# Gathering the sink columns on VectorE instead of ScalarE, in the attention stage of a fused kernel

## The chip, the core and the metric

The kernel runs on one NeuronCore of a Trainium2 chip. The metric is the device time of one execution in microseconds (us). The engines are TensorE (PE in the profile, its weight loads PEld), VectorE (DVE), ScalarE (ACT), GpSimd (POOL) and SyncE (SP), which issues the transfers. Each runs its own list of instructions in order, and they wait for each other by semaphores.

## What is computed

Three layers in a row, for 2 sequences of 768 positions. The change touches the first alone: attention of 16 heads (2 x 8) with a window of 128 positions and 4 "sink" positions that every query may see.

```python
scores = scale * np.matmul(q, k.transpose(0, 1, 3, 2))        # 2 x 8 heads, 768 x 768, D = 64
is_sink = pos[None, :] < int(n_sink)                            # 4
rel = pos[:, None] - pos[None, :]
in_window = (rel >= 0) & (rel < int(window))                    # 128
scores = np.where(is_sink | in_window, scores, -1000000000.0)
a = np.exp(scores - np.max(scores, axis=-1, keepdims=True))
a = a / (np.sum(a, axis=-1, keepdims=True) + 1e-09)
return np.matmul(a, v)
```

Behind it come a causal attention of four experts of which two count for each position, and a gated layer with a mix over the positions. They follow when all heads are done.

## The kernel before

A head's 768 queries are T = 6 tiles of 128. A query tile t sees the key tile before it, its own, and the 4 sinks, so its scores are one tile of WIN = 260 columns: 128, then 4 sinks, then 128 (for t = 0 only the last 132). The 16 heads use two sets of buffers in turn (s = 0 for even heads, 1 for odd). In one "step" of a head, `pe_step`, `act_step` and `dve_step` each do the later half of the work of that head and the first half of the next head's. The loops of the engines hold two steps, one for each s; heads 0 and 1 and the last two stand outside of them. I call the place between the two steps the middle of the body, and the place where the loop turns its edge.

First half, for head + 1 in the step of head: TensorE scores a tile (`score_tile`, two matmuls with kS as keys and qH, qL as queries); VectorE adds the mask, scales and takes the row minimum of the negated scores (`mask_tile`, SM and NM, one custom instruction and a short one that reads its accumulator); ScalarE takes the exponential and its row sum (`exp_tile`, Pa and RS). SM has a ring of three, so a mask waits for the exponential three tiles back.

Second half, for head: TensorE turns Pa in three groups (`turn_group`); ScalarE copies groups 0 and 2 out of PSUM and VectorE group 1 (`copy_group`, PTa); TensorE multiplies them by va (`weigh_group`). The sink columns go another way: `gather_sinks` copies the 4 sink columns of all six tiles, out of Pa, three times into one tile `sinks` of 128 x 96 (72 columns are written), TensorE turns that (`turn_sinks`), VectorE writes it to PS in a rounded and a rest part (`copy_sinks`), and TensorE multiplies PS by vs (`weigh_sinks`), which ends the head's sum. Then VectorE adds epsilon to the row sums and inverts them (`invert_sums`, a TENSOR_SCALAR and a RECIPROCAL on RI, 128 x 6), and in the next step multiplies the head's sum by them (`normalise`, X).

The gather before is ScalarE's, behind the last exponential of a head and ahead of the copy of group 0 in the next step. TensorE's order in a step is: score 0, turn group 0, score 1, turn group 1, turn the sinks, score 2, turn group 2, weigh group 0, scores 3 and 4, weigh group 1, score 5, weigh group 2, weigh the sinks.

GpSimd works beside them, once a pair of heads for each: it splits the queries of a later head (`split_queries`: qH, then qL, which waits for qH), lays out the sinks' values (`lay_out_sinks`: vs, which waits for `weigh_sinks` of an earlier head), and splits a strip of weights for the next layer (`split_strip`: wbH, then wbL). In the order of its loop: qH and qL of the even head, vs of the even head, qH and qL of the odd head, wbH and wbL, vs of the odd head. So the vs that follows an even step, in the middle of the body, has qH, qL, wbH and wbL behind it, and the vs that follows an odd step, at the edge, has qH and qL of the next turn. SyncE loads keys, queries and values a pair ahead.

Of the kernel before, what the change touches and what calls it, by code (L numbers as in the profile page):

```python
# [19 lines left out]
ACT = mybir.ActivationFunctionType  # L20
# [3 lines left out]
P = 128  # L24
B, H, S, D = 2, 8, 768, 64
T = S // P
SINK, WINDOW = 4, 128
# [12 lines left out]
BLK = P + SINK  # L40
# [58 lines left out]
def fused_attention_experts_gated(nc, qT, kT, v, vsink, vdiag, w_b, w_in, g_ln, w_sgT, b_sg, w_out, out):  # L99
    ctx = ExitStack()  # L100
    with ctx:
        def sb(name, shape, dt=F32, stack=ctx):
            return stack.enter_context(nc.sbuf_tensor(name, shape, dt))

        def sem(name):
            return ctx.enter_context(nc.semaphore(name))
# [26 lines left out]
        with ExitStack() as st:  # L133
# [5 lines left out]
            Pa = [sb(f"Pa{s}", [P, T, WIN], F32, st) for s in range(2)]  # L139
            SM = [sb(f"SM{s}", [P, WIN], F32, st) for s in range(RING)]  # L140
            PTa = [sb(f"PTa{s}", [P, BANK], F32, st) for s in range(2)]
            sinks = [sb(f"sinks{s}", [P, SROWS], F32, st) for s in range(2)]
# [24 lines left out]
        with ExitStack() as st:  # L167
# [14 lines left out]
        s_ = {n: sem(n) for n in (  # L182

            "consts", "pool_step",

            "q_split", "k_high", "k_split", "scored", "masked", "expd", "turned", "turned_in_act", "turned_in_dve",
            "sinks_gathered", "sinks_turned", "sinks_high", "sinks_in", "sv_in", "sv_high", "sv_low", "vs_ready",
            "weighed", "summed", "x_ready", "dve_step", "wb_split", "wo_split", "dve_chain",

            "dve_tick", "pool_tick",  # L190
# [194 lines left out]
        def _(act):  # L385
# [7 lines left out]
            def exp_tile(s, head, t, again):  # L393
                n = T * head + t
                act.wait_ge(s_["masked"], n + 1)
                if again and t == 0:
                    act.wait_ge(s_["turned"], GROUPS * (head - 1))
                    act.wait_ge(s_["sinks_gathered"], head - 1)
                    act.wait_ge(s_["dve_step"], 2 * head - 3)
                a = P if t == 0 else 0  # L400
                nc.scalar.activation(Pa[s][:, t, a:WIN], SM[t % RING][:, a:WIN], ACT.Exp, bias=NM[:, s, t:t + 1], scale=-1.0,  # L401
                                     accum_out=RS[:, s, t:t + 1]).then_inc(s_["expd"], 1)

            def gather_sinks(s, head, again):

                act.wait_ge(s_["expd"], T * (head + 1))
                if again:
                    act.wait_ge(s_["sinks_turned"], head - 1)
                nc.scalar.activation(sinks[s][:, :].rearrange("p (k n) -> p k n", k=3)[:, :, 0:T * SINK].rearrange("p k (t c) -> p k t c", t=T),
                                     Pa[s][:, :, P:BLK].unsqueeze(1).broadcast_to((P, 3, T, SINK)), ACT.Copy)\  # L410
                    .then_inc(s_["sinks_gathered"], 1)

            def copy_group(s, head, g, again):
                act.wait_ge(s_["turned"], GROUPS * head + g + 1)
                if again or g:
                    act.wait_ge(s_["weighed"], GROUPS * head + g - 1)
                m, a = (s + g) % 2, P if g == 0 else 0
                nc.scalar.activation(PTa[m][:, a:], banks[:, 4 + m, a:], ACT.Copy).then_inc(s_["turned_in_act"], 1)

            def x_high(b, t):  # L420

                act.wait_ge(s_["x_turned"], T * b + t + 1)
                nc.scalar.activation(xH[:, :, t * P:(t + 1) * P], banks[:, X_BANKS[t % RING], :].rearrange("p (k n) -> p k n", k=KT),
                                     ACT.Copy).then_inc(s_["x_high"], 1)

            def act_step(s, head, again, keys, nxt):

                copy_group(s, head, 0, again)
                for t in range(T):
                    if nxt:  # L430
                        exp_tile(1 - s, head + 1, t, again or s)
                    else:
                        x_high(0, t)
                    if t == 0 and keys is not None:
                        high_keys(s, head + 2, keys, True)
                    if t == 2:
                        copy_group(s, head, 2, again)
                if nxt:
                    gather_sinks(1 - s, head + 1, again or s)

            high_keys(0, 0, 0, False)
            high_keys(1, 1, 0, False)
            for t in range(T):
# [1 line left out]
                    act.wait_ge(s_["sv_in"], 32)  # L445
                    nc.scalar.activation(sv[:, :], sv_raw[:, :], ACT.Copy).then_inc(s_["sv_high"], 1)
                exp_tile(0, 0, t, False)
            gather_sinks(0, 0, False)
            act_step(0, 0, False, 1, True)
            act_step(1, 1, True, 1, True)  # L450
            with act.Fori(1, PAIRS - 1) as i:
# [28 lines left out]
            for b in range(B):  # L480
                for n, (kind, j, g) in enumerate(PROJ_ORDER):
                    wait("projected", PROJ * b + n + 1)
                    c = slice(g * G3 * P, (g + 1) * G3 * P)
# [37 lines left out]
            for b in range(B):  # L521
                for t in range(T):
                    n = T * b + t
# [11 lines left out]
                for t in range(T):  # L535
                    n = T * b + t
# [9 lines left out]
        def _(dve):  # L546
# [21 lines left out]
            def copy_group(s, head, again):  # L568
# [3 lines left out]
                m = (s + 1) % 2  # L572
                nc.vector.tensor_copy(PTa[m][:, :], banks[:, 4 + m, :]).then_inc(s_["turned_in_dve"], 1)  # L573

            def copy_sinks(head, again):
                dve.wait_ge(s_["sinks_turned"], head + 1)
                if again:
                    dve.wait_ge(s_["summed"], head)
                nc.vector.tensor_copy(PS[:, :], banks[0:SROWS, 2, 0:P]).then_inc(s_["sinks_high"], 1)
                dve.wait_ge(s_["sinks_high"], head + 1)  # L580
                low = slice(64, 64 + T * SINK)
                nc.vector.tensor_tensor(PS[low, :], banks[low, 2, 0:P], PS[low, :].bitcast(F32), ALU.subtract)\
                    .then_inc(s_["sinks_in"], 1)
# [9 lines left out]
            def normalise(s, head, turn):  # L593
                dve.wait_ge(s_["dve_step"], 2 * head + 2)
                dve.wait_ge(s_["summed"], head + 1)
                at = bass.ds(turn * T * P, T * P)
                nc.vector.tensor_tensor(X[:, at].rearrange("p (t n) -> p t n", t=T)[:, :, s * D:(s + 1) * D],
                                        banks[:, 6 + s, 0:T * D].rearrange("p (t d) -> p t d", t=T),
                                        RI[:, :].unsqueeze(2).broadcast_to((P, T, D)), ALU.mult).then_inc(s_["x_ready"], 1)
# [9 lines left out]
            def dve_step(s, head, before, again, keys, nxt):  # L609

                for t in range(T):
                    if nxt:
                        mask_tile(1 - s, head + 1, t, True)
                    if t == 0 and before is not None:
                        normalise(1 - s, head - 1, before)
                    if t == 2:
                        copy_group(s, head, again)
                    if t == 2 and keys:
                        low_keys(s, head + 2)
                    if t == 3:  # L620
                        copy_sinks(head, again)
                    if not nxt:
                        x_low(0, t)
                invert_sums(s, head, again)
# [101 lines left out]
            for b in range(B):  # L726
                for n, (kind, j, g) in enumerate(PROJ_ORDER):
                    if kind == "kq":
                        wait("proj_high", PROJ * b + n + 1)
                        c = slice(g * G3 * P, (g + 1) * G3 * P)  # L730
# [43 lines left out]
            for b in range(B):  # L774
# [4 lines left out]
                for t in range(T):  # L779
                    n = T * b + t  # L780
# [25 lines left out]
                for t in range(T):  # L806
                    n = T * b + t
# [362 lines left out]
```

## Time and profile before

| | us |
|---|---|
| median of 3 runs | 448.91 (448.79 to 448.92) |
| the profiled execution | 448.91, of which the span of the trace is 446.7 |
| busy in the span: PE, PEld | 418.4, 368.7 |
| busy: DVE, ACT, POOL | 269.4, 211.1, 130.2 |
| mean granted clock of TensorE | 0.992 of full speed |

The attention stage fills about the first 120 us of the span, the rest belongs to the other two layers. "Busy" is the time for which an instruction's record is open, so an instruction that stands and waits for something inside itself counts as busy. The records are given as start and length in us from the span's start; a line number such as L589 is that of the kernel printed above. "Idle before" and its releaser stand in brackets at the end of a row where an engine waited.

### The profile page before, as it was taken

To read this page: it belongs to the slowest core of one execution; us is meant where nothing else is said; L and a number is where in the kernel's file an instruction comes from. 1 tells how busy PE (TensorE), PEld (TensorE's weight loads), DVE (VectorE), ACT (ScalarE), POOL (GpSimd) and SP (SyncE) were. 2 spreads that over 40 slices of the span, in tenths; PEclk is the share of its full clock that TensorE was granted. 3 is DMA by queue.
4 is the path that set the end of the run, shared out by engine and by line. 5 is a ranking of instruction groups with operands and counts; after the bars stand their busy time and mean duration, and the time that the engine had idled before them with its cause. 6 is when DMAs were issued, how large, how long until landed. Compare 5 with 4: busy or idle time off the path is not lost.

```text
span 446.7 us, 8137 instructions
## 1 busy us (share of the span) xinstructions
PE 418.4 (94%) x2608; PEld 368.7 (83%) x2608; DVE 269.4 (60%) x687; ACT 211.1 (47%) x545; POOL 130.2 (29%) x144
## 2 busy tenths in 40 slices
PE   0899899989999999989998998999999999999997
PEld 0787788878999999869997997888888888888885
DVE  0899999999838775640879653277423335652322
ACT  2777777787646655444774653434210114331010
POOL 7877676685673000000037400232000000000000
PEclk9999999999999999989999998999999999999999
DMA  8876576571432000000003300100001010000011
GB/s 192 200 198 155 143 186 172 144 183 46 122 104 73 0 1 2 0 1 1 0 25 104 87 1 0 25 24 1 0 0 49 23 72 0 1 0 0 30 42 70
DMA packets 14156, 27.72 MB, mean 62 GB/s; under 512 B 2256, under 2 KB 5328, under 8 KB 14128
## 3 DMA queue, kind: packets, MB, share of 16 engines
q1 hardware_dynamic: 14128, 27.35, 23.1%
q8 instruction: 17, 0.28, 0.3%
q14 instruction: 11, 0.09, 0.1%
HBM read 24.20 MB, written 3.15 MB: 61 GB/s over the span
## 4 chain that ended last, share of the span: by engine, by line
PE 74%; DVE 10%; issue 7%; ACT 6%; DMA 1%; POOL 1%; DVEq 0%; SPq 0%; ACTq 0%; POOLq 0%
PE banks L826 13%; PE banks L828 13%; PE banks L827 13%; PE banks L1098 11%; PE banks L1000 7%; PE banks L978 4%; PE banks L989 4%; ACT Pa L401 3%; PE banks L877 3%; DVE kS L553 3%; DVE RI L589 2%; DVE SM L564 2%; PE banks L841 2%; PE banks L857 2%; PE banks L892 1%
## 5 line engine op out<-in xcount | busy, mean ns | idle before, releaser
L401 ACT ACTIVATE Pa<-SM,NM 128x260 f32<-128x260 f32 (+1 forms) x96 | 46.7, 487 | 22.8 <-DVE NM L564 22.4
L877 PE MATMUL banks<-va,PTa 128*128 128x64 f32 x352 | 46.0, 272 | 3.8 <-DVE PTa L573 3.3
L877 PEld LDWEIGHTS banks<-va,PTa 128*128 128x128 f32 x352 | 43.1, 191 | 6.5 <-DVE PTa L573 6.5
L841 PE MATMUL banks<-kS,qH 128*128 128x260 f32 x96 | 34.8, 367 | 13.2 <-POOL qL L321 10.8
L1000 PE MATMUL banks<-vg,PTb 128*128 128x64 f32 x336 | 44.6, 267 | 1.0 <-DVE Y L679 1.0
L1000 PEld LDWEIGHTS banks<-vg,PTb 128*128 128x128 f32 x336 | 42.2, 191 | 1.9 <-issue 1.4
L470 ACT ACTIVATE Pb<-Pb,NM 128x128 f32<-128x128 f32 (+5 forms) x48 | 31.9, 664 | 22.3 <-DVE NM L665 22.1
L564 DVE CUSTOM_DVE_ANT_0 SM<-banks,win 128x260 f32<-128x260 f32 (+1 forms) x96 | 36.4, 403 | 6.2 <-PE banks L841 3.4
L539 ACT ACTIVATE gH<-banks 128x512 fp32r<-128x512 f32 x12 | 7.2, 600 | 68.4 <-PE banks L1118 68.4
L826 PE MATMUL banks<-w_inH,x2H 128*128 128x512 f32 x96 | 38.1, 397 | 0.0
L828 PE MATMUL banks<-w_inH,x2L 128*128 128x512 f32 x96 | 37.5, 391 | 0.0
L827 PE MATMUL banks<-w_inL,x2H 128*128 128x512 f32 x96 | 37.4, 390 | 0.0
L374 POOL TENSOR_TENSOR rstd<-vare,minus_half 128x1 f32<-128x1 f32 x12 | 6.6, 553 | 98.7 <-DVE vare L787 98.7
L665 DVE CUSTOM_DVE_ANT_0 Pb<-banks,causal 128x128 f32<-128x128 f32 (+5 forms) x48 | 29.4, 620 | 7.6 <-PE banks L978 7.4
L841 PEld LDWEIGHTS banks<-kS,qH 128*128 128x128 f32 x96 | 19.1, 199 | 17.1 <-issue 10.5
L321 POOL TENSOR_TENSOR qL<-qd,qH 128x768 fp32r<-128x768 f32 x16 | 31.3, 1958 | 1.3
L796 DVE SCALAR_TENSOR_TENSOR Gd<-banks,b_all,U 128x512 f32<-128x512 f32 x12 | 9.0, 751 | 37.2 <-PE banks L1098 37.2
L360 POOL TENSOR_SCALAR w_sgH_first<-raw 128x512 fp32r<-128x512 f32 x6 | 3.7, 622 | 94.3 <-PE banks L828 92.0
L989 PE MATMUL banks<-ident,Pb 128*128 128x128 f32 x168 | 29.7, 278 | 0.9 <-ACT Pb L470 0.6
L1098 PE MATMUL banks<-vnH,w_sgL 128*128 128x512 f32 x72 | 28.3, 393 | 0.0
L857 PE MATMUL banks<-ident,Pa 128*128 128x128 f32 x176 | 27.5, 275 | 0.6 <-ACT Pa L401 0.3
L841 PE MATMUL banks<-kS,qL 128*128 128x260 f32 x96 | 27.6, 291 | 0.0
(150 smaller groups left out, 1107.2 us busy)
## 6 DMA issues: line engine op xcount, KB each, us to landing
kd<-in_kT SPq DMA_DIRECT2D x32, 198.0 KB, 3.7
qd<-in_qT SPq DMA_DIRECT2D x32, 192.0 KB, 3.9
va<-in_v SPq DMA_DIRECT2D x16, 192.0 KB, 3.5
out<-O SPq DMA_DIRECT2D x12, 256.0 KB, 2.0
raw<-in_w_sgT SPq DMA_DIRECT2D x9, 256.0 KB, 2.6
raw<-in_w_in SPq DMA_DIRECT2D x8, 256.0 KB, 2.7
raw<-in_w_b SPq DMA_DIRECT2D x8, 193.0 KB, 3.7
raw<-in_w_out SPq DMA_DIRECT2D x4, 256.0 KB, 2.8
```

What stands on the lines that cost most here:

```text
L401: nc.scalar.activation(Pa[s][:, t, a:WIN], SM[t % RING][:, a:WIN], ACT.Exp, bias=NM[:, s, t:t + 1], scale=-1.0, accum_out=RS[:, s, t:t + 1 ...
L470: nc.scalar.activation(Pb[n % RING][:, 0:w], Pb[n % RING][:, 0:w], ACT.Exp, bias=NM[:, e % 2, t:t + 1], scale=-1.0, accum_out=RS[:, e % 2, ...
L564: nc.vector.tensor_tensor_reduce(out=SM[t % RING][:, a:WIN], in0=banks[:, A_BANKS[t % RING], 0:WIN - a], in1=m[:, :], scale=-SCALE, scalar ...
L826: nc.tensor.matmul(out, aH, bH, start=(n == 0), stop=False)
L827: nc.tensor.matmul(out, aH, bL, start=False, stop=False)
L828: last = nc.tensor.matmul(out, aL, bH, start=False, stop=(n == k - 1))
L841: last = nc.tensor.matmul(banks[:, A_BANKS[t % RING], 0:WIN], q[s][:, t * P:(t + 1) * P], kS[s][:, c:c + WIN], start=first_, stop=not first_)
L857: last = nc.tensor.transpose(banks[:, m, j * P:(j + 1) * P], Pa[s][:, t, own * BLK:own * BLK + P], ident[:, :])
L877: last = nc.tensor.matmul(banks[:, 6 + s, t * D:(t + 1) * D], PTa[m][:, j * P:(j + 1) * P], va[s][:, t - 1 + own, :], start=(t == 0), stop ...
L989: last = nc.tensor.transpose(banks[:, TURN_BANKS[m % (E * CHUNK_N) % RING], j * P:(j + 1) * P], Pb[n % RING][:, (j0 + j) * P:(j0 + j + 1) ...
L1000: last = nc.tensor.matmul(banks[:, SUM_BANK, t * D:(t + 1) * D], PTb[m % RING][:, j * P:(j + 1) * P], vg[:, j0 + j, e * D:(e + 1) * D], st ...
L1098: last = nc.tensor.matmul(banks[:, 6 + n % 2, :], a, x[:, s, :], start=(s == 0 and k == 0), stop=(s == T - 1 and k == 2))
```

## The change

`gather_sinks` moves from ScalarE to VectorE. It is the same copy with the same operands and the same two waits (all six exponentials of the head, and the turn of the sinks two heads back), now `tensor_copy` in place of an activation with Copy. On ScalarE it stood at the end of the step before (behind the last exponential of the head). On VectorE it stands in the head's own step, behind the mask of tile 0 of the next head and ahead of `normalise`. Nothing else is changed.

```diff
@@ scalar
-            def gather_sinks(s, head, again):
-                act.wait_ge(s_["expd"], T * (head + 1))
-                if again:
-                    act.wait_ge(s_["sinks_turned"], head - 1)
-                nc.scalar.activation(sinks[s][:, :].rearrange("p (k n) -> p k n", k=3)[:, :, 0:T * SINK].rearrange("p k (t c) -> p k t c", t=T),
-                                     Pa[s][:, :, P:BLK].unsqueeze(1).broadcast_to((P, 3, T, SINK)), ACT.Copy)\
-                    .then_inc(s_["sinks_gathered"], 1)
...
-                if nxt:
-                    gather_sinks(1 - s, head + 1, again or s)
...
-            gather_sinks(0, 0, False)
@@ vector
+            def gather_sinks(s, head, again):
+                dve.wait_ge(s_["expd"], T * (head + 1))
+                if again:
+                    dve.wait_ge(s_["sinks_turned"], head - 1)
+                nc.vector.tensor_copy(sinks[s][:, :].rearrange("p (k n) -> p k n", k=3)[:, :, 0:T * SINK].rearrange("p k (t c) -> p k t c", t=T),
+                                      Pa[s][:, :, P:BLK].unsqueeze(1).broadcast_to((P, 3, T, SINK)))\
+                    .then_inc(s_["sinks_gathered"], 1)
...
                     if nxt:
                         mask_tile(1 - s, head + 1, t, True)
-                    if t == 0 and before is not None:
-                        normalise(1 - s, head - 1, before)
+                    if t == 0:
+
+                        gather_sinks(s, head, again and not (isinstance(head, int) and head == 1))
+                        if before is not None:
+                            normalise(1 - s, head - 1, before)
```

On VectorE, at the top of the loop's body, the order was this (L564 is a mask with its accumulator, L597 `normalise`; REGISTER_ALU and the bare ISA rows set registers):

```order
L564 ISA SM,NM<-banks,win 128x132 [waits expd]
L564 ISA NM 128x1
L594 ISA
L597 ISA [waits summed,dve_step]
L597 TENSOR_TENSOR X<-banks,RI 128x6x64
L558 REGISTER_ALU
L560 REGISTER_ALU [waits scored]
L564 ISA SM,NM<-banks,win 128x260 [waits expd]
```

And with the change it is this (L552 is the mask, L567 the gather, L593 `normalise`):

```order
L552 ISA SM,NM<-banks,win 128x132 [waits expd]
L552 ISA NM 128x1
L566 REGISTER_ALU [waits expd]
L567 COPY sinks<-Pa 128x3x24 [waits sinks_turned]
L590 ISA
L593 ISA [waits summed,dve_step]
L593 TENSOR_TENSOR X<-banks,RI 128x6x64
L546 REGISTER_ALU
L548 REGISTER_ALU [waits scored]
L552 ISA SM,NM<-banks,win 128x260 [waits expd]
```

The COPY of 3 x 24 elements came in between the first mask and X, and everything behind it in the step moved back by one.

On ScalarE, from the last exponential of a step (L401) over the middle of the body to the copy of group 0 (L418), it was this:

```order
L401 ACTIVATE Pa,RS<-SM,NM 128x260 [waits masked]
L406 ISA
L409 ACTIVATE sinks<-Pa 128x3x24 [waits sinks_turned,expd]
L414 ISA
L416 REGISTER_ALU [waits turned]
L418 ACTIVATE PTa<-banks 128x384 [waits weighed]
L395 REGISTER_ALU
```

And with the change (L409 is now the copy of group 0):

```order
L401 ACTIVATE Pa,RS<-SM,NM 128x260 [waits masked]
L405 ISA
L407 REGISTER_ALU [waits turned]
L409 ACTIVATE PTa<-banks 128x384 [waits weighed]
L395 ISA
```

The copy of group 0 now follows the last exponential directly. The orders of TensorE, GpSimd and SyncE are as they were.

## Rows read from the trace of the kernel before

**Rows 1.** Table by windows: busy us (x instructions) of each engine.

```profile
core 0: us, PE busy (x) PEld busy (x) DVE busy (x) ACT busy (x) POOL busy (x), PEclk, DMA share, GB/s
59.00:73.00 14.00, 12.71 (x98) 11.15 (x96) 12.83 (x40) 10.77 (x36) 9.38 (x9) 1.00 0.74 182
```

**Rows 2.** Timeline, one pair of heads: start, length, engine, line, operation.

```profile
61.97 0.83 POOL L336 TENSOR_TENSOR vs<-sv,diag 96x384 fp32r<-96x384 f32 x1 [2.97 <-PE banks L884]
...
61.99 1.63 DVE L589 TENSOR_SCALAR RI<-RS 128x6 f32<-128x6 f32 x1
...
62.77 0.83 POOL L319 TENSOR_SCALAR qH<-qd 128x768 fp32r<-128x768 f32 x1
...
63.68 1.83 POOL L321 TENSOR_TENSOR qL<-qd,qH 128x768 fp32r<-128x768 f32 x1
...
64.40 0.56 DVE L597 TENSOR_TENSOR X<-banks,RI 128x384 f32 x1
...
64.87 0.42 DVE L564 CUSTOM_DVE_ANT_0 SM<-banks,win 128x260 f32<-128x260 f32 x1
...
65.48 0.82 POOL L326 TENSOR_TENSOR wbH<-raw,ones 128x386 f32 x1
...
66.28 0.98 DVE L553 TENSOR_TENSOR kS<-kd,kS 64x792 fp32r<-64x792 f32 x1
...
67.54 1.00 PE L877 MATMUL banks<-va,PTa 128*128 128x64 f32 x8
...
68.35 0.42 PE L884 MATMUL banks<-vs,PS 96*128 96x384 f32 x1
...
68.95 0.83 POOL L336 TENSOR_TENSOR vs<-sv,diag 96x384 fp32r<-96x384 f32 x1 [0.82 <-PE banks L884]
...
68.98 0.82 DVE L589 TENSOR_SCALAR RI<-RS 128x6 f32<-128x6 f32 x1
...
70.66 1.83 POOL L321 TENSOR_TENSOR qL<-qd,qH 128x768 fp32r<-128x768 f32 x1
```

**Rows 3.** Instructions of one line: count, ns min/median/max, first and last start.

```profile
L589 DVE TENSOR_SCALAR RI<-RS x16: 163/825/1633, 21.8 to 122.0; 128x6 f32<-128x6 f32 x16
...
L409 ACT ACTIVATE sinks<-Pa x16: 262/263/266, 16.4 to 115.6; 128x72 f32<-128x72 f32 x16
```

**Rows 4.** Timeline of VectorE and of GpSimd at the stage's start.

```profile
18.55 1.50 DVE L553 TENSOR_TENSOR kS<-kd,kS 64x792 fp32r<-64x792 f32 x1
...
18.39 0.83 POOL L319 TENSOR_SCALAR qH<-qd 128x768 fp32r<-128x768 f32 x1
19.30 2.43 POOL L321 TENSOR_TENSOR qL<-qd,qH 128x768 fp32r<-128x768 f32 x1
```

**Rows 5.** Timeline of TensorE in the first two steps.

```profile
16.70 0.32 PE L864 MATMUL banks<-ident,sinks 128*96 128x128 f32 x1 [0.63 <-ACT sinks L409]
...
16.97 0.28 PE L841 MATMUL banks<-kS,qL 128*128 128x260 f32 x1
...
18.22 0.36 PE L841 MATMUL banks<-kS,qH 128*128 128x260 f32 x1
...
19.91 1.06 PE L877 MATMUL banks<-va,PTa 128*128 128x64 f32 x8
...
23.38 0.28 PE L841 MATMUL banks<-kS,qL 128*128 128x260 f32 x1
23.50 0.60 PE L857 MATMUL banks<-ident,Pa 128*128 128x128 f32 x4
...
24.52 0.37 PE L841 MATMUL banks<-kS,qH 128*128 128x260 f32 x1
```

**Rows 6.** Timeline of GpSimd and of VectorE at the stage's end.

```profile
109.44 0.83 POOL L336 TENSOR_TENSOR vs<-sv,diag 96x384 fp32r<-96x384 f32 x1 [0.96 <-PE banks L884]
...
121.95 1.33 POOL L362 TENSOR_TENSOR w_inL<-raw,w_inH 128x512 fp32r<-128x512 f32 x1
...
121.97 0.16 DVE L589 TENSOR_SCALAR RI<-RS 128x6 f32<-128x6 f32 x1
```

## What I expect of the change

> **What bounds the kernel now.** I read the table by windows first. In the attention stage, here a stretch of 14 us, the records cover 12.71 us of TensorE and 12.83 us of VectorE but 10.77 us of ScalarE [rows 1]. ScalarE, which gives the gather away, has slack; VectorE, which takes it, has none. So I read VectorE and GpSimd side by side. A head's step is 6.5 to 7 us: the `vs` tile of GpSimd starts at 61.97 (I call this moment V) and at 68.95 [rows 2]; V comes at 68.95 and 109.44 with three pairs of heads between them, 40.49 / 3 = 13.50 us a pair [rows 2, 6].
>
> The reader should look at the one TENSOR_SCALAR of each step, RI<-RS on six numbers. Its shortest record is 163 ns, its median 825, its longest 1633 [rows 3]. In the middle of the loop body it starts 0.02 us after `vs` and ends at 63.62, just behind the end of qH (63.60); at the loop's edge it starts 0.03 after `vs` and ends at 69.80, just behind the end of `vs` (69.78) [rows 2]. It is a small SBUF-to-SBUF operation that is held while GpSimd runs; in the first place it is not let in between `vs` and qH, which follow without a gap, but in the short gap ahead of qL it is. TENSOR_TENSOR kS<-kd,kS, whose inputs are both in SBUF, is held too: 1.50 us beside qH instead of 0.98 [rows 2, 4]. The operations that read PSUM (SM, X, PTa) are not.
>
> **The gather leaves ScalarE.** 16 ACTIVATEs of 263 ns [rows 3], about 4.2 us of an engine that is idle 3 us in 14 [rows 1]. TensorE needs the result only at its turn of the sinks. Value on the path: 0 for certain; 0.26 a head would be the most.
>
> **The gather enters VectorE** as a COPY from SBUF to SBUF, behind the first mask of a step and ahead of X<-banks,RI. Alone it should take between the 0.16 of the TENSOR_SCALAR and the 0.26 that ScalarE took; I take 0.2. What counts is when GpSimd lets it go. The nearest row to it is the TENSOR_SCALAR (one source, SBUF to SBUF, float32), so I take it as held in the same way, and ending 0.04 behind the GpSimd operation. Queued behind it are X, the masks, PTa, kS; TensorE stands at the turn of the sinks and cannot score the next tile.
>
> The Trainium skill ("SBUF — State Buffer", Who interferes with whom) has this as an exclusive lock on a port pair that GpSimd shares with copies and tensor_scalar in their two-port mode; "Vector Engine (DVE) Microarchitecture Reference", Performance modes, asks for an outermost dimension that is even, or odd and equal on both sides. By these two the copy (outermost 3 and 3) takes the lock and waits. No run here has yet shown it for this shape. The lengths of the TENSOR_SCALAR agree with the lock.
>
> Let G be the end of a gather. I replay one step from it.
> - VectorE: X started at 64.40 and the next TENSOR_SCALAR at 68.98, 4.58 later. X starts about 0.08 before the end of what is ahead of it, as the mask at 64.87 does before X's end at 64.96 [rows 2]. So the TENSOR_SCALAR comes at G+4.50.
> - TensorE, which was waiting: 0.05 to start the turn; 0.27 to the second matmul of the next score (16.70 to 16.97); 0.12 (23.38 to 23.50); 1.02 to the score of tile 3 (23.50 to 24.52); 1.69 from that score to the last group of weighings (18.22 to 19.91, another step); 0.81 to the sinks' matmul (67.54 to 68.35): 3.96. Then 0.60 to `vs` (68.35 to 68.95) [rows 2, 5]. V = G+4.56.
>
> So the order of two starts decides. Before, `vs` was first by 0.02 to 0.04 each time and VectorE was held 0.8 or 1.6 us. Now the TENSOR_SCALAR should be first, by 0.06. The closest tie in the trace, at 121.95 and 121.97, went to VectorE (its TENSOR_SCALAR is 0.16 us long, although GpSimd's record starts 0.02 earlier) [rows 6]. Being first costs GpSimd 0.10 and frees VectorE of its hold; the gather then takes that hold over: it waits for the end of qH, 1.63 behind V (62.77+0.83-61.97). G to G is 4.56+0.10+1.63+0.04 = **6.33 us** (a "won" step).
>
> Behind a won step in the middle of the body GpSimd is late: qL begins at G+0.06 (63.68 against 63.62) and takes 1.83, wbH follows at G+1.86 (it starts 0.03 before qL's end, 65.48 against 65.51) and lasts until G+2.68. kS would start at G+1.80 (66.28-64.40-0.08), and is caught behind wbH: it ends at 2.68+0.83 = 3.51 instead of 2.78. From kS's end to V are 1.69 (67.26 to 68.95), so V = G+5.20, TensorE is no longer late, and `vs` is first again ("lost"). At the edge the gather then finds qL running until V+3.54 (72.49-68.95), and ends at V+3.58: G to G is 5.20+3.58 = **8.78**. Behind that GpSimd is idle, and the next step is won. A pair takes 6.33+8.78 = 15.11 instead of 13.50.
>
> **The sum.** The first gather meets GpSimd at work; kS of that step comes behind qL, which starts at 19.30, takes 1.83 without hindrance and 0.83 more for kS: 21.96 instead of 20.05 [rows 2, 4], 1.9 us. V is then 23.6, this race is lost as before, and the gather of head 1 is held behind qL and wbH, 4.37 us from V (66.30-61.97+0.04): G = 28.0. A won step: 34.3. Five pairs of 15.11: 109.9. A won step: 116.2. V of the last edge: 121.4, against 109.44 before [rows 6]. That is +12.0; two more gathers behind which GpSimd has nothing of the loop to do add 0.2. The profiled execution took 448.91 (span 446.7), the same as the median of the runs, 448.91; so 448.9+12.2 = **461.1 us**. The stages after attention move as a whole; SP's queue loses nothing, since `kd` and `qd` land in 4 us of a turn of 13 or more.
>
> **Rivals.**
> 1. `vs` is first in every step: it needs the 0.08 overlap of X to be missing behind a held copy, which makes the TENSOR_SCALAR's start G+4.61, 0.05 after V. Then a middle step is 4.37+4.58 = 8.95 and an edge step 3.58+4.58 = 8.16: 17.1 a pair. From G = 28.0: 36.1, five pairs: 121.6, V at 135.2: +26 us, **474.9**. For it: all 14 races before went to GpSimd, and the margin is 0.06. Against it: every operation in the trace that waits for nothing starts before its forerunner's end.
> 2. The races are won and kS slips in ahead of wbH. It asks for the port 0.15 after its start (0.98 less 0.83), at about G+1.95, and wbH starts at G+1.86. Then each step is 6.33, a pair 12.66; 34.3+63.3+6.33+4.56 = 108.5, +0.2: **448.2**, no slower than before. It decides whether GpSimd hands the port to its next operation: between `vs` and qH in the middle of the body it does, at the edge it does not [rows 2]. wbH resembles the first.
 It then costs 0.2, TensorE is late all the same and wins the middle race; but kS comes early against qL and wbH and gives it back, ending near V+5.2, so V' = V+6.9; the edge step after it is V' + 2.1 + 4.56 = 6.7. A pair is 13.6: **449 to 450**. The Trainium skill ("VectorE: DVE Perf Modes", the errata section) would make such a copy an estimated (58+36)/0.96 = 98 ns, cheaper than the 263 of ScalarE; by that alone 16 of them would cost at most 1.6 us.
>
> **How the numbers follow.** The forecast with one race won and one lost in a pair (or the two the other way round: 6.33 and 4.56+4.37 = 8.93, 15.26 a pair and 462 by the same sum): 0.52. Rival 1: 0.24. Rival 2: 0.10. Rival 3: 0.10; 0.04 for others. To hold 8 in 10 the range takes the forecast, rival 1 and one of the others: 448 to 476. A measurement tells 0.2% (0.9 us) from no change. Slower: 0.52+0.24, and 0.06 out of the rest: 0.82. Same: 0.11. Faster: 0.07.
>
> **What would show it.** In the changed kernel sinks<-Pa on VectorE should be 1 to 2 us long, not 0.2, and end just behind qH in one step of a pair and behind qL in the other. RI<-RS should be near 0.16 in the steps that follow the long gathers and near 0.8 at the edge. kS in the step after a won middle race should be 1.7, and TensorE's wait before the turn of the sinks should be the longest of the stage. Steps of 6.3 and 8.8 confirm the sum; of 8.2 and 9.0, rival 1. Records of 0.2 for the gather, or a pair near 12.7, would prove the forecast wrong. So would a lower granted clock in this stage, for which no row speaks [rows 1].

## The result, and the profile after

| | before | changed |
|---|---|---|
| median | 448.85 us (448.74 to 448.92) | 470.02 us (469.19 to 471.52) |
| ratio | | 1.0487, 95% interval 1.0444 to 1.0529 |
| span of the profiled execution | 446.7 us | 465.9 us |

The change costs 21.2 us by the medians, 19.2 by the two traces. The forecast was 461.1, a cost of 12.2, with a range up to 476. It had the direction and the place right, and the cost too small by 9 us. Three further executions of the changed kernel took 469.57 to 473.79 us.

First the lengths of the two small copies in the changed kernel, by line: L567 is the gather, L585 the TENSOR_SCALAR on RI, the twin of L589 in [rows 3].

```profile
L567 DVE COPY sinks<-Pa x16: 303/1122/1827, 17.1 to 137.9; 128x72 f32<-128x72 f32 x16
...
L585 DVE TENSOR_SCALAR RI<-RS x16: 166/168/1636, 23.9 to 144.4; 128x6 f32<-128x6 f32 x16
```

The gather's median is 1122 ns where ScalarE's was 263, and never under 303. The TENSOR_SCALAR's median fell from 825 to 168: in most steps the hold went over from the one to the other. The next rows are a pair of heads of the changed kernel, VectorE first and then GpSimd from the timeline.

```profile
57.94 1.12 DVE L567 COPY sinks<-Pa 128x72 f32<-128x72 f32 x1
61.02 1.55 DVE L541 TENSOR_TENSOR kS<-kd,kS 64x792 fp32r<-64x792 f32 x1
64.29 0.80 DVE L585 TENSOR_SCALAR RI<-RS 128x6 f32<-128x6 f32 x1
66.01 1.82 DVE L567 COPY sinks<-Pa 128x72 f32<-128x72 f32 x1
...
73.39 0.17 DVE L585 TENSOR_SCALAR RI<-RS 128x6 f32<-128x6 f32 x1
74.63 1.12 DVE L567 COPY sinks<-Pa 128x72 f32<-128x72 f32 x1
```

```profile
58.17 0.83 POOL L319 TENSOR_SCALAR qH<-qd 128x768 fp32r<-128x768 f32 x1
59.09 1.85 POOL L321 TENSOR_TENSOR qL<-qd,qH 128x768 fp32r<-128x768 f32 x1
60.89 0.84 POOL L326 TENSOR_TENSOR wbH<-raw,ones 128x386 f32 x1
...
64.23 0.83 POOL L336 TENSOR_TENSOR vs<-sv,diag 96x384 fp32r<-96x384 f32 x1 [0.94 <-PE banks L883]
...
65.95 1.82 POOL L321 TENSOR_TENSOR qL<-qd,qH 128x768 fp32r<-128x768 f32 x1
...
74.07 0.83 POOL L336 TENSOR_TENSOR vs<-sv,diag 96x384 fp32r<-96x384 f32 x1 [6.31 <-PE banks L883]
```

Read the ends against each other. The gather from 57.94 ends at 59.06, behind qH's 59.00. kS from 61.02 ends at 62.57, caught behind wbH (61.73). TENSOR_SCALAR comes 0.06 behind `vs` and is held 0.80. The gather from 66.01 ends at 67.83, behind qL's 67.77. That is the alternation of the forecast. But from that gather's end (67.83) to the next `vs` (74.07) are 6.24 us where the forecast had 4.66. The next row, of TensorE (its turn of the sinks), and the table by windows show why.

```profile
67.98 0.42 PE L863 MATMUL banks<-ident,sinks 128*96 128x128 f32 x1 [2.18 <-DVE sinks L567]
```

```profile
core 0: us, PE busy (x) PEld busy (x) DVE busy (x) ACT busy (x) POOL busy (x), PEclk, DMA share, GB/s
68.00:69.00 1.00, 1.00 (x5) 1.00 (x6) 0.63 (x3) 0.33 (x1) 0.00 (x0) 0.50 0.85 286
69.00:70.00 1.00, 1.00 (x7) 1.00 (x6) 0.95 (x3) 0.74 (x4) 0.00 (x0) 0.50 0.01 5
70.00:71.00 1.00, 1.00 (x7) 1.00 (x7) 0.97 (x2) 0.17 (x3) 0.00 (x0) 0.50 0.00 0
71.00:72.00 1.00, 1.00 (x9) 1.00 (x9) 0.49 (x4) 0.56 (x1) 0.00 (x0) 0.81 0.00 0
72.00:73.00 1.00, 1.00 (x11) 1.00 (x11) 0.93 (x6) 0.60 (x2) 0.00 (x0) 1.00 0.46 92
```

TensorE stood for 2.2 us in front of the turn of the sinks; then its granted clock was at half of full speed (1.2 instead of 2.4 GHz) for some 3.5 us, and it started 5 to 7 matmuls in a microsecond instead of 11. Over the stage:

```profile
20.00:132.00 112.00, 94.77 (x639) 90.68 (x638) 93.21 (x272) 68.15 (x203) 60.94 (x54) 0.83 0.47 120
```

The mean granted clock is 0.83; before it was 1.00 in every window of the stage. The last `vs` at a loop's edge stands at 132.14 in this trace:

```profile
132.14 0.83 POOL L336 TENSOR_TENSOR vs<-sv,diag 96x384 fp32r<-96x384 f32 x1 [4.43 <-PE banks L883]
```

Before it was at 109.44 [rows 6]: the stage lost 22.7 us. The spans differ by 19.2, so 3.5 us came back behind it. The first of these rows is of before, the second of the changed kernel, each for the layer of the experts:

```profile
120.00:280.00 160.00, 154.56 (x1093) 144.84 (x1093) 98.06 (x263) 86.41 (x218) 31.45 (x33) 0.98 0.11 30
...
144.00:300.00 156.00, 150.84 (x1082) 141.78 (x1081) 98.06 (x261) 86.28 (x218) 30.11 (x32) 1.00 0.11 30
```

Before, the profiled execution had a short dip of the clock there (0.98), which the changed kernel's did not. It explains the 3.5 us by an estimate: the clock is 0.91 in the windows from 180 to 200 and from 260 to 280 us, and 0.09 of these 40 us are 3.6. Also, executions of the kernel before that ran beside the experiments below took 445.1 to 448.9 us, with medians near 447.1. Against those the change costs some 23 us, which fits the 22.7 of the stage.

### The profile page after: what moved, and what is told of

The parts are those of the page before. It is cut to its first block, busy times and chain, and to the rows that moved or that the text cites. A ratio compares the mean times of both kernels' runs of the same rounds, so it can differ in the third digit from the quotient of the medians.

```text
span 465.9 us, 8125 instructions
## 1 busy us (share of the span) xinstructions
PE 427.5 (92%) x2608; PEld 383.6 (82%) x2608; DVE 281.2 (60%) x703; ACT 209.7 (45%) x529; POOL 127.9 (27%) x144
## 4 chain that ended last, share of the span: by engine, by line
PE 77%; DVE 10%; issue 8%; ACT 2%; DVEq 1%; DMA 1%; POOL 1%; SPq 0%; ACTq 0%; POOLq 0%
PE banks L825 12%; PE banks L827 12%; PE banks L826 12%; PE banks L1097 11%; PE banks L999 6%; PE banks L876 6%; PE banks L977 4%; PE banks L840 4%; PE banks L988 4%; PE banks L856 2%; DVE sinks L567 2%; DVE SM L552 2%; DVE RI L585 1%; PE banks L891 1%; PE banks L945 1%
## 5 line engine op out<-in xcount | busy, mean ns | idle before, releaser
L401 ACT ACTIVATE Pa<-SM,NM 128x260 f32<-128x260 f32 (+1 forms) x96 | 47.1, 491 | 36.5 <-DVE NM L552 36.4
L876 PE MATMUL banks<-va,PTa 128*128 128x64 f32 x352 | 52.5, 299 | 0.0
L876 PEld LDWEIGHTS banks<-va,PTa 128*128 128x128 f32 x352 | 51.9, 224 | 0.0
L552 DVE CUSTOM_DVE_ANT_0 SM<-banks,win 128x260 f32<-128x260 f32 (+1 forms) x96 | 37.9, 404 | 19.9 <-PE banks L840 13.9
L840 PE MATMUL banks<-kS,qH 128*128 128x260 f32 x96 | 38.2, 402 | 11.5 <-POOL qL L321 10.4
L840 PEld LDWEIGHTS banks<-kS,qH 128*128 128x128 f32 x96 | 22.9, 239 | 13.2 <-issue 10.4
L856 PE MATMUL banks<-ident,Pa 128*128 128x128 f32 x176 | 32.3, 310 | 0.0
L840 PE MATMUL banks<-kS,qL 128*128 128x260 f32 x96 | 31.0, 327 | 0.0
```

The lines of the kernel that those rows point to most:

```text
L552: nc.vector.tensor_tensor_reduce(out=SM[t % RING][:, a:WIN], in0=banks[:, A_BANKS[t % RING], 0:WIN - a], in1=m[:, :], scale=-SCALE, scalar ...
L840: last = nc.tensor.matmul(banks[:, A_BANKS[t % RING], 0:WIN], q[s][:, t * P:(t + 1) * P], kS[s][:, c:c + WIN], start=first_, stop=not first_)
L856: last = nc.tensor.transpose(banks[:, m, j * P:(j + 1) * P], Pa[s][:, t, own * BLK:own * BLK + P], ident[:, :])
L876: last = nc.tensor.matmul(banks[:, 6 + s, t * D:(t + 1) * D], PTa[m][:, j * P:(j + 1) * P], va[s][:, t - 1 + own, :], start=(t == 0), stop ...
```

## The experiments

Each ran beside the kernel before on one chip; its time in those batches was 447.06, 447.09 and 447.01 us, and the ratios are against that.

**1. The gather as tensor_reduce.** The same data in the same place on VectorE, by another instruction.

```diff
-                nc.vector.tensor_copy(sinks[s]..., Pa[s][:, :, P:BLK].unsqueeze(1).broadcast_to((P, 3, T, SINK)))
+                nc.vector.tensor_reduce(sinks[s]..., Pa[s][:, :, P:BLK].unsqueeze(1).broadcast_to((P, 3, T, SINK)).unsqueeze(4),
+                                        axis=AX.X, op=ALU.max)
```

> The changed kernel with the gather written as tensor_reduce (maximum over an axis of one element) in place of tensor_copy: same place, same engine, same data. Hold theory (the copy is held because its two-port form shares SBUF access with GpSimd): the gather is 0.2 to 0.3 us long in every step, TensorE's wait before the turn of the sinks stays under 1 us, the granted clock of the attention stage stays 1.00, and the time is 446 to 452 us. Rival, placement (the gather is late because it stands behind a mask on the fullest engine, whatever its form): the gather's record is still 1 us and more, or it is short and the time is still near 470 us.

449.18 us, ratio 1.0032 (1.0004 to 1.0059). The timeline of VectorE and, below it, of GpSimd:

```profile
65.05 0.22 DVE L567 TENSOR_REDUCE sinks<-Pa 128x72 f32<-128x72 f32 x1
...
64.48 1.84 POOL L321 TENSOR_TENSOR qL<-qd,qH 128x768 fp32r<-128x768 f32 x1
```

It runs in the middle of qL and takes 0.22 us; all 16 take 222 to 230 ns. The Trainium skill says of tensor_reduce that it has no two-port mode on trn2 and never contends ("SBUF — State Buffer", Who interferes with whom); these rows agree. So all but 1.4 us (by the ratio, with an interval of 0.2 to 2.6; 2.1 by the medians) are the hold of the copy and what it drags along, and the rest is the place and the engine. TensorE's wait before the turn of the sinks was not under 1 us as expected: in the steady part it was 1.5 us in the middle steps and 0.5 to 0.6 at the edge, and the granted clock of the stage stayed at 1.00.

**2. Work for TensorE while it waits.** Results unused.

```diff
+                for _ in range(16 if s == 0 else 4):
+                    nc.tensor.transpose(banks[:, 2, 2 * P:3 * P], ident[:, :], ident[:, :])
                 pe.wait_ge(s_["sinks_gathered"], head + 1)
```

> The changed kernel with TensorE turning the identity into unused PSUM columns ahead of its wait for the gather, 16 times in even steps and 4 times in odd ones, results unused. Clock theory (about 1.6 us of each long-wait step are matmuls at half clock behind the wait): granted clock 1.00 throughout the stage, from the end of a held gather to the next vs 4.6 us instead of 6.2, a pair 15.1 instead of 16.7, the time 459 to 463 us. Rival (all of the loss is the hold itself and its queue; the low clock is hidden behind VectorE): granted clock 1.00 too, but the time stays within 468 to 473 us.

485.1 us, ratio 1.0875 (1.0815 to 1.0935), above both ranges. I had given the long filler to the steps that wait long in the changed kernel, and the filler moved the long wait into the others. TensorE's timeline has both kinds, ahead of the turn (L865):

```profile
33.00 1.91 PE L863 MATMUL banks<-ident 128*128 128x128 f32 x16
34.75 0.27 PE L865 MATMUL banks<-ident,sinks 128*96 128x128 f32 x1
...
60.37 0.60 PE L863 MATMUL banks<-ident 128*128 128x128 f32 x4
63.07 0.32 PE L865 MATMUL banks<-ident,sinks 128*96 128x128 f32 x1 [2.09 <-DVE sinks L567]
```

And the windows behind each:

```profile
36.00:38.00 2.00, 2.00 (x19) 2.00 (x19) 1.94 (x5) 1.04 (x3) 0.00 (x0) 1.00 0.24 76
...
66.00:68.00 2.00, 2.00 (x11) 2.00 (x11) 1.29 (x6) 1.21 (x4) 0.00 (x0) 0.50 0.26 60
```

Behind the 16 without a wait the clock stays at 1.00; behind the 4 and a wait of 2.09 us it is at 0.50. The kernel itself is slow because its 16 fillers then also run at half clock, beyond the wait: at 72.30 they take 2.97 us instead of the 1.91 above, and the turn of the sinks comes at 75.10, 3.09 us behind the end of its gather (72.01).

**3. Filler in every step.** Here 14 turns in each step, and of a tile of Pa in place of the identity.

```diff
+                for _ in range(14):
+                    nc.tensor.transpose(banks[:, 2, 2 * P:3 * P], Pa[s][:, 0, P + SINK:WIN], ident[:, :])
                 pe.wait_ge(s_["sinks_gathered"], head + 1)
```

> The changed kernel with 14 turns of a tile of Pa into unused PSUM columns, results unused, ahead of TensorE's wait for the gather in every step (before, 16 and 4 of them, and the clock fell behind the steps that had 4). Clock theory: granted clock 1.00 in the whole stage; from the end of a gather to the next vs 4.6 to 5.2 us everywhere; gathers still held, 1.1 to 1.8 us; a pair about 16 us or less, the time 458 to 467 us, that is less than the changed kernel in spite of added work. Rival (the low clock is no cause of time): 469 us or more.

469.43 us, ratio 1.0495 (1.0460 to 1.0530), and the clock of the stage is 1.00. The cause of the low clock is confirmed, and its price is not: the time is that of the changed kernel. The filler itself does not hide a gain within the loop, since TensorE still waits 0.6 to 1.1 us behind it for every held gather there. The pair shows what came in place of the low clock. VectorE, then GpSimd, then TensorE (the turn of the sinks and the end of the next score) by the timeline:

```profile
57.57 1.30 DVE L567 COPY sinks<-Pa 128x72 f32<-128x72 f32 x1
...
59.24 0.41 DVE L552 CUSTOM_DVE_ANT_0 SM<-banks,win 128x260 f32<-128x260 f32 x1
...
59.69 0.43 DVE L552 CUSTOM_DVE_ANT_0 SM<-banks,win 128x260 f32<-128x260 f32 x1
...
63.47 0.84 DVE L585 TENSOR_SCALAR RI<-RS 128x6 f32<-128x6 f32 x1
...
55.28 0.83 POOL L336 TENSOR_TENSOR vs<-sv,diag 96x384 fp32r<-96x384 f32 x1 [4.65 <-PE banks L885]
...
56.99 1.81 POOL L321 TENSOR_TENSOR qL<-qd,qH 128x768 fp32r<-128x768 f32 x1
58.76 0.83 POOL L326 TENSOR_TENSOR wbH<-raw,ones 128x386 f32 x1
...
63.45 0.83 POOL L336 TENSOR_TENSOR vs<-sv,diag 96x384 fp32r<-96x384 f32 x1 [2.82 <-PE banks L885]
...
58.92 0.31 PE L865 MATMUL banks<-ident,sinks 128*96 128x128 f32 x1 [0.97 <-DVE sinks L567]
...
59.19 0.28 PE L840 MATMUL banks<-kS,qL 128*128 128x260 f32 x1
```

`vs` is first in every step, by 0.01 to 0.05 us (0.02 here). From the step at 38.89 to the one at 120.78 the two holds follow each other every time; `vs` to gather's end takes 3.59 (55.28 to 58.87), and a pair 16.35 us (55.28 to 71.63). That is rival 1 of the prediction, only with 3.6 in place of 4.37 in the middle. In the changed kernel a slow TensorE makes `vs` late and lets the TENSOR_SCALAR win every other time: the low clock costs 1.66 us in a step (6.24 from a gather's end to the next `vs` instead of 4.58) and saves 1.91 at its end (1.68 instead of 3.59), but then kS is caught behind wbH, which gives back 0.59 (5.17 to the next `vs` instead of 4.58). A pair there takes 16.69 (64.23 to 80.92).

The last `vs` of the loop stands at 128.99, 3.1 us earlier than in the changed kernel. From it to the last TENSOR_SCALAR of the stage are 15.1 us instead of 12.3: the last two gathers are not held (0.20 and 0.32 us), and there the filler does stand in the path. So the whole time understates a little what the clock costs; within the loop it is some 3 of the 22.7 us.

**4. GpSimd splits the strip first.**

```diff
-                split_queries(1, 2 * i + 1, i, True)
                 split_strip(i, bass.ds(i * WB_STEP, WB_STEP))
+                split_queries(1, 2 * i + 1, i, True)
```

> The changed kernel with GpSimd splitting the weight strip ahead of the odd head's queries instead of behind them; all work is kept. Theory of the alternating steps (kS is caught behind wbH, that makes VectorE late, vs is first, and the next gather waits for the end of qL): kS is 0.98 us long in every step of the loop, the TENSOR_SCALAR on RI is 0.17 in every step, every gather ends with the second GpSimd operation of its burst, 0.8 to 1.2 us long, TensorE waits about 1 us and the clock stays at 1.00; a pair takes 12.7 to 13.2 us and the time is 446 to 453 us. Rival (the gathers at the edge are held behind qL in any case): the gathers of even heads are still 1.8 us, 466 us or more.

460.63 us, ratio 1.0317 (1.0273 to 1.0360): 9.4 us better than the changed kernel, and outside of both ranges, at least 7.6 us above that of the theory and 5 below that of the rival. Holds moved again. Rows of VectorE and of GpSimd:

```profile
69.35 0.57 DVE L567 COPY sinks<-Pa 128x72 f32<-128x72 f32 x1
71.89 1.53 DVE L541 TENSOR_TENSOR kS<-kd,kS 64x792 fp32r<-64x792 f32 x1
...
68.86 1.00 POOL L329 TENSOR_TENSOR wbL<-raw,wbH 128x386 f32 x1 [0.17 <-POOL wbH L326]
...
70.75 1.84 POOL L321 TENSOR_TENSOR qL<-qd,qH 128x768 fp32r<-128x768 f32 x1
```

In the steady middle steps of the changed kernel the TENSOR_SCALAR was not held, the gather took 1.12 us and kS 1.53 to 1.55, behind wbH. Here the TENSOR_SCALAR ahead of the gather is held (67.09, 1.63 us), the gather takes 0.57, and kS is caught all the same, 1.53 us, now behind qL. In this kernel, too, the order of GpSimd's work changed who was held, and not that someone was.

**5 to 8. Without the add.** The TENSOR_SCALAR adds 1e-9 to row sums of at least 1, which changes no float32, and can go.

```diff
-                nc.vector.tensor_scalar(RI[:, :], RS[:, s, :], EPS_SUM, None, ALU.add).then_inc(s_["dve_step"], 1)
-                dve.wait_ge(s_["dve_step"], 2 * head + 1)
-                nc.vector.reciprocal(RI[:, :], RI[:, :]).then_inc(s_["dve_step"], 1)
+                nc.vector.reciprocal(RI[:, :], RS[:, s, :]).then_inc(s_["dve_step"], 2)
```

In the kernel before:

> The kernel before with the epsilon's TENSOR_SCALAR on the row sums left out (the row sums are at least 1, where adding 1e-9 changes no float32), so that the reciprocal reads them directly. Hold theory: VectorE loses no 0.8 and 1.6 us at the start of vs; kS then comes early and is held behind qL and wbH instead, which gives most of it back: about 13.0 us a pair instead of 13.5, 443 to 447 us. Rival (the holds add up and nothing takes their place): 14 steps times 1.1 us less, 433 to 436 us.

439.25 us, ratio 0.9820 (0.9793 to 0.9846). It lies between the two ranges and in neither: some of the hold moves to kS (median 1.21 us instead of 0.98), the rest is gained, 7.8 us. VectorE, then GpSimd, in a middle step:

```profile
62.09 1.33 DVE L553 TENSOR_TENSOR kS<-kd,kS 64x792 fp32r<-64x792 f32 x1
...
60.72 1.86 POOL L321 TENSOR_TENSOR qL<-qd,qH 128x768 fp32r<-128x768 f32 x1
62.52 1.59 POOL L326 TENSOR_TENSOR wbH<-raw,ones 128x386 f32 x1
```

kS waits behind qL and is let in at its end (62.58), although wbH's record has begun; it ends 0.84 later, and this time it is wbH that is longer, 1.59 us instead of 0.83. It is so in all seven middle steps.

In the changed kernel:

> The changed kernel without the epsilon's TENSOR_SCALAR on the row sums (adding 1e-9 changes none of them). Theory that the gather's hold alone sets the step: the gather ends with the same GpSimd operation whether something was held ahead of it or not, so records of it grow by what the TENSOR_SCALAR lost, and the time stays at 465 to 471 us. Rival (the two holds add up): about 0.8 us less in each of 7 steps and more, 455 to 461 us.

449.24 us, ratio 1.0049 (1.0023 to 1.0075): 20.8 us better than the changed kernel, and below both ranges. VectorE, then GpSimd:

```profile
63.40 0.18 DVE L585 RECIPROCAL RI<-RS 128x6 f32<-128x6 f32 x1
64.30 0.76 DVE L567 COPY sinks<-Pa 128x72 f32<-128x72 f32 x1 [0.22 <-ACT Pa L401]
...
63.38 0.83 POOL L336 TENSOR_TENSOR vs<-sv,diag 96x384 fp32r<-96x384 f32 x1 [2.77 <-PE banks L881]
64.18 0.83 POOL L319 TENSOR_SCALAR qH<-qd 128x768 fp32r<-128x768 f32 x1
65.09 1.85 POOL L321 TENSOR_TENSOR qL<-qd,qH 128x768 fp32r<-128x768 f32 x1
```

`vs` is first by 0.02, but the reciprocal is not held by it (0.18 us). So the gather comes 0.9 us behind V, is still ahead of qL, and ends at 65.06 behind qH, 1.68 from V. In experiment 3 the held TENSOR_SCALAR brings the gather 2.3 us behind V, into qL, and it ends at 3.6. I had expected it to end with the same operation either way. It does not: with both operations in place one burst of GpSimd holds VectorE twice, since the first hold delays the second operation past the gap that it could have used.

With the gather as tensor_reduce, and then with TensorE's turn of the sinks moved two slots back as well:

> The gather on VectorE as tensor_reduce, and the epsilon's TENSOR_SCALAR left out, so that neither is held. Against the kernel with the gather on ScalarE and the same omission, 439.25 us, it tells what the move itself is worth. Theory (VectorE's place is late: TensorE waits about 1 us a step for the gather): 441 to 447 us. Rival (the 0.26 us that ScalarE saves ahead of its first copy pays): 434 to 438 us.

```diff
                     elif t == 1:
                         turn_group(s, head, 1, again)
-                        turn_sinks(s, head, again)
...
                     elif t == 3:
-                        pass
+                        turn_sinks(s, head, again)
```

> As the kernel before this one (gather as tensor_reduce on VectorE, no epsilon add), with TensorE turning the sinks two slots later, behind the score of tile 3. Theory (TensorE's wait for the gather is what the move costs once nothing is held): TensorE no longer waits for the gather and the time falls to 433 to 440 us. Rival (VectorE's own list with kS held is the bound): within 1 us of the kernel before this one.

441.89 us, ratio 0.9870 (0.9838 to 0.9901), and 438.79 us, ratio 0.9806 (0.9779 to 0.9834). The first lies in the range of the theory and says that the move by itself costs 2.6 us (against 439.25) where neither the gather nor the add is held. The second takes off 3.1, and no wait of TensorE for the gather is left among its waits. What the move costs without a hold is that TensorE stands for a result that comes later; the twin below tests that.

**9 and 10. Twins on ScalarE.**

> The kernel before (gather on ScalarE) without the epsilon's TENSOR_SCALAR, and with TensorE's turn of the sinks two slots later. It is the twin of the 438.79 us kernel, which gathers on VectorE by tensor_reduce. Theory (with nothing held and no wait for the gather, the engine that gathers matters little, and the 0.2 us on the fuller VectorE cost more than ScalarE's 0.26): 436 to 438.8 us, no slower than its twin. Rival (the move off ScalarE pays once it isn't held): 439.5 us or more.

439.06 us, ratio 0.9820 (0.9776 to 0.9864), 0.3 above the range of the theory: against 438.79 no difference that can be told, and none against 439.25 either, the same kernel with the turn in its old place. So the later turn is worth its 3.1 us only where TensorE waits for VectorE's gather. Once neither the gather nor the add is held and TensorE does not wait for the gather, its engine makes no difference here. kS is still held in both (median 1.27 us in the one and 1.56 in this one, where 0.98 is its length unheld).

> The kernel before without the epsilon's TENSOR_SCALAR, and with kS<-kd,kS behind the copy of the sinks instead of ahead of the mask of tile 3, so that it starts 0.9 us later, when qL has ended. Theory (the 0.35 us for which kS is held behind qL are on the path): kS 0.98 us in steps at the edge, still held behind wbH in the middle, 435 to 438.5 us. Rival (TensorE's own work is the bound once the first hold is gone): 438.8 to 440 us.

```diff
-                    if t == 2 and keys:
-                        low_keys(s, head + 2)
                     if t == 3:
                         copy_sinks(head, again)
+                        if keys:
+                            low_keys(s, head + 2)
```

440.75 us, ratio 0.9848 (0.9808 to 0.9887), above both ranges. Behind the first step kS is no longer held (0.96 to 0.97 us), in the middle steps as well, and the time is not better. By the traces the last `vs` of the loop is at 102.35 against 101.94 with kS in its old place, so this way of freeing kS gains nothing in the stage; whether the hold of kS is on the path at all is not shown by it, since kS also comes later. Its profiled execution took 437.14 at a mean granted clock of 1.000, its other four 440.7 to 440.8 at 0.992.

The table puts the six together (us):

| gather | with the add | without |
|---|---|---|
| ScalarE | 447.1 to 448.9 | 439.3 |
| VectorE, copy | 470.0 | 449.2 |
| VectorE, tensor_reduce | 449.2 | 441.9 |

The held add alone costs 7.3 to 7.8, the held copy alone 7.3, both together 28 (470.0 against 441.9): they are not two costs but a queue. The fastest kernels, 438.79 us with the gather on VectorE and 439.06 and 439.25 with it on ScalarE, can't be told apart and are below both of the comparison.

## Why the prediction was right and wrong

**Right.** The copy is held (experiment 1). ScalarE's saved 0.26 us brings nothing that shows (439.06 against 438.79 us). The replay behind a gather in the middle: kS ends 3.51 us behind G (forecast 3.51), `vs` comes at G+5.17 (5.20), and the edge's gather ends 3.60 behind V (3.58). X starts 0.07 to 0.08 before the copy's end, as forecast.

**Wrong: the race at full clock.** The forecast put the TENSOR_SCALAR at G+4.50, 0.06 ahead of `vs`. Experiment 3 has G = 58.87, V = G+4.58 (forecast 4.56), and the TENSOR_SCALAR at G+4.60. The changed kernel has two such steps of its own, where the clock had been at full speed since the gather before; VectorE, then GpSimd:

```profile
38.94 1.64 DVE L585 TENSOR_SCALAR RI<-RS 128x6 f32<-128x6 f32 x1
...
38.92 0.83 POOL L336 TENSOR_TENSOR vs<-sv,diag 96x384 fp32r<-96x384 f32 x1 [2.77 <-PE banks L883]
```

Here, and at 122.36 against 122.39, `vs` is first, and the gather ends 3.59 and 3.58 behind it. What failed is the step "X started at 64.40 and the next TENSOR_SCALAR at 68.98, 4.58 later" carried over: in it no mask waits for its score. Behind a gather TensorE starts late, and the mask of tile 2 has to wait for it. From one mask to the next are 0.45 us in experiment 3 (59.24 to 59.69), and before they were 0.34, by VectorE's timeline:

```profile
64.87 0.42 DVE L564 CUSTOM_DVE_ANT_0 SM<-banks,win 128x260 f32<-128x260 f32 x1
...
65.21 0.42 DVE L564 CUSTOM_DVE_ANT_0 SM<-banks,win 128x260 f32<-128x260 f32 x1
```

In experiment 3 the score of tile 2 ends at 59.47 and its mask starts 0.22 later; in the changed kernel the same 0.22 lie between a score's end (71.40) and a mask that the trace shows waiting for it (71.62). So the lateness is 0.1 us against a margin of 0.06: VectorE could not get ahead of the engine that feeds it. The margin itself would have been enough: at the edge of experiment 4 the TENSOR_SCALAR starts 0.04 to 0.05 ahead of `vs` (60.70 against 60.74) and is not held, 0.17 us. With a clock at full speed rival 1 would have been the likeliest. Two smaller points belong here: before, `vs` was first by 0.02 to 0.06, not 0.02 to 0.04; and the kS that was forecast at 1.7 us took 1.53, because it too started 0.18 later than forecast and ended at the same time.

**Wrong by omission: the clock.** It was named as what would make the forecast wrong, and as something "for which no row speaks". The prediction had TensorE standing at every held gather of the edge and priced that at the wait alone. The "won" step took 6.24 + 1.68 = 7.92 us where 6.33 was forecast. The last `vs` was forecast at 121.4 and came at 132.14, 10.7 us later. Up to the end of the third gather the sum holds (34.27, forecast 34.3), by luck in part: the first `vs` came 1.9 late at half clock, and a race won because of that and a gather that found a gap (33.97, 0.30 us) made up for it. The next ten steps took 16.69 us a pair (34.27 to 117.72) instead of 15.11, that is 7.9 us. The last two steps took 1.9 more by a race lost at full clock (122.36) and 1.0 more behind it at half clock. But experiment 3 shows that most of this is not an added cost of the clock: without the low clock the lost race takes its place, at 16.35 us a pair.

**Right number, wrong reason: the middle steps.** They were "won" in most of the steady part of the stage as forecast (73.39 against 74.07), not by the 0.06 us of the sum but by 0.68, because TensorE was at half clock.

**Wrong: 4.37.** Rival 1 and the start had the middle gather held behind qL and wbH. It ends 0.07 behind qL (58.87 against 58.80 in experiment 3), although wbH's record has begun at 58.76, just as kS is let in between the two in the seven middle steps of the kernel before without the add. Between `vs` and qH, whose records overlap in the same way, the TENSOR_SCALAR was kept out in all seven middle steps before. What differs between the two places is open. It was not on the forecast's main path except at the start.

**Rival 3**, the copy that is not held, has its twin in experiment 1, and there its number came out and its mechanism did not: 449.2, forecast 449 to 450, but against 447.1 beside it and not 448.9. TensorE is late as it said, but the middle race is still lost (62.77 against 62.79, the TENSOR_SCALAR held 1.64 us) and kS is not caught (0.98 us); a pair takes 13.78 us (62.77 to 76.55), forecast 13.6. The price of 98 ns that it has from the Trainium skill ("VectorE: DVE Perf Modes", the errata section) halves the 72 elements for a mode that this rival denies; without the halving the same row gives an estimated (58+72)/0.96 = 135 ns. Measured, the tensor_reduce took 222 to 230 ns and the shortest copies in the traces 0.20 to 0.21 us, so the measurement decides against both.

## What to carry to other kernels

Before a small operation is moved to another engine, look how long its nearest relative there takes at its shortest and at its longest record: here a factor of ten between them (163 to 1633 ns) was a hold by a third engine, and a second operation of the same kind in the same burst did not share that hold but stood behind it. Take the form that is not held (here a tensor_reduce for the copy, and no add at all), and ask who now waits for the result: once neither was held, that wait was what the move cost. When a replay ends in a race of a few hundredths of a microsecond, follow every wait between the two engines before calling it, and give the other outcome as much weight.

## What the runs showed of the hardware

- In the stage of the changed kernel the granted clock fell from full to half (2.4 to 1.2 GHz) six times, each time at a turn of the sinks for which TensorE had stood 1.9 to 2.6 us, or up to 1.6 us behind it: three times for 3.4 us and three times for 6.8 to 10.2. In experiment 2 the same followed six waits of 2.1 us (3.4 to 10.7 us at half clock), but a seventh, of 2.15 us at 27.32, was followed by full clock. In experiment 4 waits of 1.86 and 1.87 us were followed by half clock, and others of 1.7 to 1.85 us were not. With unused turns ahead of the wait in every step the clock stayed at 1.00 (experiment 3).
- A held operation of VectorE ends a fixed time behind the GpSimd operation that held it: kS 0.83 to 0.86 us, the TENSOR_SCALAR 0.02 to 0.03, the gather 0.04 to 0.08.
- Near ties between `vs` and the TENSOR_SCALAR went to the record that started first: to `vs` when it was 0.01 to 0.06 us ahead (14 of 14 before, and each such tie of experiments 1 to 4), to the TENSOR_SCALAR when it was 0.04 to 0.05 ahead (4 of 4 at the edge in experiment 4).
- An operation of VectorE that waited behind qL was let in at qL's end although wbH's record had begun (kS without the add, the gather in experiment 3). One that waited behind `vs` in the middle of the body was let in only after qH.
- Executions of one kernel differ by dips of the clock: 437.14 us at a mean of 1.000 and 440.7 to 440.8 at 0.992 in experiment 10. In the profiled execution of the kernel before the dips lie behind the stage (180 to 200 and 260 to 280 us).
